# Second products of a gated MLP one slot later, in a fused attention + mixture-of-experts + MLP kernel on one core

## The reference

```python
x = _attn_ref(...)                      # 2 x 768 tokens, 512 channels, decayed linear attention
x = _moe_ref(x, domain_probs, w1, w2)   # 4 experts, 512 -> 1024 -> 512
def _moe2_ref(x, w_in, w_out):          # 1536 tokens, 512 -> 2048 -> 512
    h = x @ w_in
    g = h * np.cos(h)
    return (g @ w_out).astype(np.float32)
```

## Time and profile before

| | |
|---|---|
| median of 3 runs | 833.54 us (833.54 to 835.22) |
| the profiled execution, its own time | 833.52 us |
| its span | 831.6 us |
| PE busy | 804.2 us, 97% |
| DVE, ACT, POOL busy | 597.0, 334.4, 400.1 us |
| granted clock of TensorE, mean | 0.991 |
| MLP: first matmul (L1395) to the span's end | 539.0 to 831.6 us |

### The profile page before, as it was taken

How to read it: one execution, slowest core, us unless ns; L and a number is a source line. 1 busy time by engine, 2 the same in 40 slices (tenths; PEclk the granted TensorE clock), 3 DMA queues, 4 the chain that set the end, 5 groups by cost and what they waited for, 6 DMA issues and landing times.

```text
span 831.6 us, 11709 instructions
## 1 busy us (share of the span) xinstructions
PE 804.2 (97%) x4362; PEld 670.8 (81%) x4362; DVE 597.0 (72%) x924; ACT 334.4 (40%) x630; POOL 400.1 (48%) x357
## 2 busy tenths in 40 slices
PE   8999999999999999999999999979989989899898
PEld 7888888888888888888888888857867768677676
DVE  6887766766766766766766766687686776867796
ACT  4653222222222232232232232365757567575653
POOL 3976343343343343343343341547776667757631
PEclk9999999999999999999999999999999999999999
DMA  9931101121101111110110110001110101010003
GB/s 326 336 129 64 39 26 39 39 64 39 39 26 38 39 64 38 39 36 30 39 38 26 39 39 26 13 26 26 38 37 27 39 13 39 13 51 26 0 4 149
DMA packets 19868, 44.85 MB, mean 54 GB/s; under 512 B 2344, under 2 KB 2392, under 8 KB 19812
## 3 DMA queue, kind: packets, MB, share of 16 engines
q1 hardware_dynamic: 19812, 44.10, 16.3%
HBM read 40.93 MB, written 3.17 MB: 53 GB/s over the span
## 4 chain that ended last, share of the span: by engine, by line
PE 69%; DVE 14%; ACT 10%; issue 4%; DMA 1%; POOL 1%; SPq 0%; ACTq 0%; DVEq 0%
PE ps L1337 31%; PE ps L1318 27%; DVE temps L1185 5%; PE ps L1402 4%; DVE temps L1179 3%; PE ps L1395 2%; ACT temps L853 2%; ACT temps L834 2%; DVE temps L1131 1%; PE ps L1285 1%; PE ps L1235 1%; DMA att<-att_in 1%; DVE x_lo L995 1%; ACT ps L812 1%; ACT w_hi L664 1%
## 5 line engine op out<-in xcount | busy, mean ns | idle before, releaser
L553 POOL TENSOR_TENSOR h_lo<-temps,h_hi 128x512 fp32r<-128x512 f32 (+1 forms) x128 | 135.1, 1057 | 295.6 <-ACT h_hi L723 295.5
L723 ACT ACTIVATE h_hi<-temps 128x512 fp32r<-128x512 f32 (+1 forms) x128 | 67.2, 525 | 337.0 <-DVE temps L1007 337.0
L990 DVE TENSOR_TENSOR y<-ps,y 128x512 f32<-128x512 f32 x180 | 123.9, 689 | 71.8 <-PE ps L1337 71.8
L1337 PE MATMUL ps<-h_hi,w_hi 128*128 128x512 f32 x384 | 150.5, 392 | 0.1
L1318 PE MATMUL ps<-x_hi,w_hi 128*128 128x512 f32 (+1 forms) x448 | 150.5, 336 | 0.1
L1318 PE MATMUL ps<-x_hi,w_lo 128*128 128x512 f32 (+1 forms) x448 | 150.6, 336 | 0.0
L1318 PE MATMUL ps<-x_lo,w_hi 128*128 128x512 f32 (+1 forms) x448 | 150.5, 336 | 0.0
L1337 PE MATMUL ps<-h_lo,w_hi 128*128 128x512 f32 x384 | 150.4, 392 | 0.0
L1337 PE MATMUL ps<-h_hi,w_lo 128*128 128x512 f32 x384 | 149.4, 389 | 0.0
L603 POOL TENSOR_TENSOR x_lo<-temps,x_hi 128x512 fp32r<-128x512 f32 x54 | 73.1, 1364 | 52.1 <-ACT x_hi L789 51.8
L1318 PEld LDWEIGHTS ps<-x_hi,w_hi 128*128 128x128 f32 x448 | 84.7, 189 | 12.8 <-DVE temps L1002 0.3
(11 more groups left out here) (111 smaller groups left out, 1404.1 us busy)
## 6 DMA issues: line engine op xcount, KB each, us to landing
w_raw<-w_in SPq DMA_DIRECT2D x96, 256.0 KB, 2.7
att<-att_in SPq DMA_DIRECT2D x24, 512.0 KB, 7.0
temps<-p_scr SPq DMA_DIRECT2D x4, 768.0 KB, 4.2
out<-y SPq DMA_DIRECT2D x12, 256.0 KB, 2.1
att<-dp_in SPq DMA_DIRECT2D x1, 24.0 KB
p_scr<-att SPq DMA_DIRECT2D x1, 24.0 KB
lam<-lam_in SPq DMA_DIRECT2D x1, 6.0 KB, 1.6
```

The source lines that it names most:

```text
L553: pool.tensor_tensor(hs_lo[side][:, f, at], ring(s, i), f32(hs_hi[side][:, f, at]), ALU.subtract).then_inc(s_hlo, 1)
L723: act.activation(hs_hi[s % SIDES][:, f, at], ring(s, i), ACT.Copy).then_inc(s_hhi, 1)
L990: dve.tensor_tensor(at, from_bank, at, ALU.add).then_inc(s_y, 1)
L1337: mm = pe.matmul(ps[:, DOWN_BANK + g % DOWN_BANKS, :], ww[:, s // SIDES % 2, f, at], hh[side][:, f, tokens], start=(f == 0 and n == 0), st ...
```

## The change

The second products of quarters 0 to 6 move one slot later on TensorE, and VectorE's taking out of their results with them, since both read `mix`. Groups 0 to 3 now stand in slot 5, groups 4 and 5 in slot 0 of the next quarter, 6 to 9 in slot 1, 10 to 13 in slot 2, 14 and 15 in slot 3, 16 and 17 in slot 4. The last quarter's groups stay; groups 16 and 17 of quarter 6 come into part 0 of slot 46, which also has the first groups of the last quarter. ScalarE's carry-ins and carry-outs, its high of the sums (from quarter 1 on), and VectorE's combinations in the last quarter move one slot later too. GpSimd's low of T1 and of the second piece of the first weights come ahead of the sums' low. No instruction is added or removed.

```diff
 def mix(v, part):
-    if v < 4:
-        return 0, ()
-    m, t = (v - 4) // 6, (v - 4) % 6
-    return m, (MIX_LAST if m == FULL else MIX)[t][part]
+    groups = []
+    if v >= 5:
+        m, t = (v - 5) // 6, (v - 5) % 6
+        if m == FULL - 1 and t == 5:
+            groups += [(m, i) for i in ((16, 17) if part == 0 else ())]
+        elif m < FULL:
+            groups += [(m, i) for i in MIX[t][part]]
+    if v >= 6 * FULL + 4:
+        groups += [(FULL, i) for i in MIX_LAST[v - 6 * FULL - 4][part]]
+    return groups
...
                     gate_low(m, 1, 1)
+                    w1_low(q + 1, 1)
+                    token_low(m, 2, t2[0])
                     w2_sums_low(m)
-                    token_low(m, 2, t2[0])
-                w1_low(q + 1, 1)
...
-                if j == 1 and m:
+                if j == 2 and m:
                     carry_in(m - 1, 14)
-                if j == 2 and m:
+                if j == 3 and m:
                     carry_in(m - 1, 16)
...
                 elif j == 3:
                     sum_high(m, 2, 0)
-                    carry_out(m, 0)
-                    carry_out(m, 1)
                 elif j == 4:
                     gate_high(m, 3, 3)
                     sum_high(m, 4, 1)
+                    carry_out(m, 0)
+                    carry_out(m, 1)
...
-                if j == 1 and m:
+                if j == 2 and m:
                     carry_out(m - 1, 14)
-                if j == 2:
+                if j == 3:
                     if m:
                         carry_out(m - 1, 16)
                     carry_in(m, 0)
                     carry_in(m, 1)
                 if m < FULL:
-                    if j == (2 if m else 1):
+                    if j == (3 if m else 1):
                         w2_sums_high(m)
...
-                if m == FULL and j == 0:
+                if m == FULL and j == 1:
...
-                if m == FULL and j == 3:
+                if m == FULL and j == 4:
                     combined(5, second_sum(N5), second_sum(N5), second_sum(N7))
                     combined(6, second_sum(N3), second_sum(N3), second_sum(N6))
```

More of the change, by code:

```diff
@@ L1098, in second @@
             def second(v, part):
-                m, groups = mix(v, part)
-                for i in groups:
+                for m, i in mix(v, part):
                     if kept(m, i) or carried(m, i):
@@ L1412, in second @@
             def second(v, part):
-                m, groups = mix(v, part)
-                q = QUARTERS + m
-                for i in groups:
+                for m, i in mix(v, part):
+                    q = QUARTERS + m
                     if m == 0 and i == 0:
```

5 lines of the change are left out of this document (3 added, 2 removed).

## The result

| | before | after |
|---|---|---|
| median | 833.84 us (832.95 to 835.22, 18 runs) | 831.38 us (828.89 to 834.78, 18 runs) |
| ratio, 95% interval | | 0.997 (0.9961 to 0.998) |
| profiled execution, its span | 833.52, 831.6 us | 832.66, 830.7 us |
| granted clock, mean | 0.991 | 0.995 |
| last matmul starts | 828.12 | 827.27 |

823.1 was forecast with a range of 812.5 to 831.0; the time lies just above the range, and nearest to rival C (831.9).

What follows compares the result with a forecast made beforehand. The chain between ScalarE and VectorE was taken to set the MLP's pace. First quarter -5.3, five steady quarters -8.0, last stretch -0.8, end +2.7 and +1.0 gave -10.4 us: 823.1 us, range 812.5 to 831.

Steps and rivals of the forecast that it cites:

- rival C: Nothing gained: the pace doesn't depend on where the carried work stands; -1.6 us, 831.9 or above, chance 0.07.
- (a): Steady quarter, end of slot 2 to L834 of slot 3: two carry-ins and the sums' high leave, one carry-in comes, -1.5 us.
- (d): Slot 5, L834 to L853: one taking out less ahead of L1185, but L1185 probably meets a GpSimd low; -0.2 us.
- (f): Slot 2: group 13's taking out comes ahead of L1185, which waits for gate 1's low anyway; 0.
- (b): Slot 3, L834 to L853: L1185 would wait for T1's low on GpSimd; +0.4 us.
- (c): L853 of slot 3 to L853 of slot 4: a carry-out, two carry-ins and the sums' high come; +0.4 us.
- Term (e): Slots 0 and 1: carry-in gone -0.5, one taking out more +0.6, a carry-out gone -0.5; together -0.4 us.
- The first quarter: L834 of slot 3 of quarter 1 comes 5.3 us earlier, at 591.4; PE allows just that, nothing left over.
- The last stretch: Slot 3 of quarter 6 to slot 3 of the last: 32.3 us for PE and one stall, not 33.1; -0.8.
- The end: Slot 46 must make the 12 matmuls that slot 4 lost, +2.7 us; the later last two combinations cost +1.0.
- A: PE becomes the bound as L1185 moves off GpSimd's lows and collisions mostly vanish; -20.9 us, 812.6, chance 0.20.
- D: Slower: T4 and L1185 of slots 4, 5 and 0 wait for whole GpSimd operations; 836.1 us, chance 0.11.

Runs made afterwards that it cites:

- experiment 1: Changed kernel with a one-element GpSimd memset between gate 5's low and the second weights' low, quarters 0 to 6: 823.52 us, ratio 0.9885.
- experiment 3: Kernel before with one VectorE instruction ahead of L1185 in slot 0, quarters 1 to 7: one-element memset 834.74 us, 128-element memset 835.39, copy from PSUM 834.83.
- experiment 5: Changed kernel with GpSimd's old order: 825.38 us; second, kernel before with GpSimd's new order alone: 838.63; changed kernel with only T1's low behind the sums' low: 823.75.
- experiment 2: Changed kernel with the same one-element GpSimd memset one place later, behind the second weights' low: 831.43 us, ratio 0.9963.
- experiment 6: First, changed kernel with the last quarter's third and fourth combinations ahead of its first group's taking out: 831.09 us; second, all four combinations plus experiment 1's memset: 822.07.

## Why the prediction was wrong, step by step

**What bounds the kernel: right.** The chain sets the pace. Slot 2 to 3 lost 1.48 us (forecast 1.5) and TensorE found its banks earlier, but the quarter became only 0.3 shorter, as much as the chain gave. TensorE's idle time is still what the chain leaves over: 3.2 us a quarter (34.5 less 31.3), where 1.9 was forecast. The two smaller stalls that stood ahead of it are gone as forecast, and the one ahead of group 8, now in slot 1's product, is there, 1.5 us instead of 1.9; a new one waits for a carry-in, 0.60 at 727.12 (TensorE's timeline, quarter 5):

```profile
717.80 0.50 PE L1409 MATMUL ps<-x_hi,h_hi 128*128 128x512 f32 x1 [1.35 <-DVE y L1127]
```

**Terms (a) to (d) and (f): right.** For (b) L1192 was to meet T1's low: it does (699.63, 1.69 long, ending 0.55 after GpSimd's L610 of 699.48 and 1.29). For (c) L842 of slot 4 was to come 3.7 after L861 of slot 3 and L861 of slot 4 6.8 after it; they came 3.67 (701.35 to 705.02) and 6.84 (708.19) after. The sums' low was to start at 3.8: it started at 3.85 (705.20).

**Term (e): this is the step that failed.** "The carry-in ahead of L834 of slot 1 has gone, -0.5" is true, as the kernels in which the race is won show (4.33). But the term let L1185 of slot 0 keep its 0.67, and said nothing of whom it meets. It meets L592 or L599 within 10 ns. +0.63 was measured where -0.5 was forecast, 1.13 a quarter, and the rows have 1.15; the 7.9 us of experiment 1 are the seven quarters of it (7 x 1.15 = 8.1). Of the 8.2 us between forecast and account, 5.7 are in the five steady quarters, 1.2 in the last stretch (forecast -0.8, measured +1.1), and 0.9 in the first (2.4 won; 3.3 with the memset, 51.41 against 54.75 from the MLP's first L834). The rest, 2.0 in the first quarter, 0.7 in the last stretch and 0.3 at the end, is below.

**The steady quarters of before: a gain that was not in the forecast.** Against all this the forecast was too modest by 2.5 in the five quarters: it took 34.8 for each quarter of before, but two of them took 36.1, those in which L1185 of slot 0 had lost its race by 0.3. The windows say why (the granted clock is the number ahead of the DMA share), before and then after:

```profile
645.00:650.00 5.00, 4.73 (x14) 3.74 (x15) 4.53 (x8) 2.79 (x5) 3.23 (x3) 0.66 0.01 2
750.00:755.00 5.00, 4.07 (x12) 3.25 (x13) 4.53 (x8) 2.60 (x6) 3.56 (x3) 0.70 0.00 0
```

```profile
645.00:650.00 5.00, 3.61 (x16) 2.61 (x15) 3.92 (x7) 2.79 (x5) 4.48 (x4) 1.00 0.01 3
```

Before, TensorE stood still for 1.82 us until 645.27, and from 646.37 on made seven steps of 0.43 instead of 0.227: the lower of its two levels, 1.2 GHz. The result that VectorE takes out just ahead of L1185 came late by that:

```profile
650.60 0.69 DVE L1120 TENSOR_TENSOR h_f<-ps,h_f 128x512 f32<-128x512 f32 x1 [0.20 <-PE ps L1402]
```

In the five profiles with TensorE's order of before (the kernel before, the three of experiment 3 and the second of experiment 5) there are eleven such stretches of 0.43 us steps behind 570 us, and eleven races of slot 0 lost by 0.27 us or more, each just behind one of them. In the nine profiles with the changed order every window of 5 us from 570 to 810 us has a clock of 1.00. So 2.6 of the 4.9 us gained in these quarters are two accidents of the kernel before that have no counterpart after the change. The prediction did not have them; it read the 0.96 of the earlier trace rows, a window that holds the first of these falls, as the slow start of quarter 0. What in the change keeps the clock up is not shown; TensorE's longest stall of 590 to 800 us is 1.4 us after it, 1.8 before.

The rest of the five quarters is chance. They were put at -1.6 each where the terms add up to -1.3, 1.5 us in all; that came true because slots 3 to 5 of quarter 1 take 11.89 and not 12.67, and slot 5 to 0 is 0.12 shorter than by term (d). And experiment 1, where the race is won, lands at 823.5 beside the 823.1 forecast in part by luck: the 2.5 us from the clock make up for most of the 3.0 that the next three paragraphs miss.

**The first quarter: the wrong bound.** "PE allows just that ... nothing is left over" took TensorE for the bound: 28.6 us for 126 matmuls and 1.6 for the slow clock make 30.2, but from TensorE's restart to L842 of slot 3 it is 33.1 (562.53 to 595.61). TensorE was at its lower level for longer than before, nine steps of 0.43 us against six. Windows before, then after, the idle time ending at 561.16 and at 562.53:

```profile
560.00:565.00 5.00, 3.84 (x10) 3.04 (x11) 3.69 (x5) 1.32 (x3) 2.39 (x3) 0.57 0.00 0
565.00:570.00 5.00, 5.00 (x24) 4.14 (x23) 2.95 (x5) 3.62 (x6) 3.35 (x3) 1.00 0.44 105
```

```profile
560.00:565.00 5.00, 2.47 (x6) 1.99 (x7) 4.93 (x6) 2.09 (x4) 2.39 (x3) 0.53 0.00 0
565.00:570.00 5.00, 5.00 (x19) 4.02 (x18) 3.61 (x5) 3.39 (x6) 5.00 (x4) 0.78 0.18 52
```

But that is not why the stretch takes 33.1. Five kernels share it and lose its race (after, experiment 2, both changed kernels of experiment 5, and the first of experiment 6); they have 9, 8, 10, 7 and 6 slow steps, the step into group 8 behind them is 1.21, 1.56, 1.02, 1.65 and 1.79 us, the shorter the more slow steps there were, and the stretch takes 33.08 to 33.13 in all five. The chain is the bound here too, and by its steps it gave less than the prediction's list has:

| from slot to slot | counted on | measured |
|---|---|---|
| 3 to 5 of quarter 0 | -1.96, two waits of ScalarE | -1.33 |
| 5 to 0 | -0.2, (d) | -0.01 |
| 0 to 1 of quarter 1 | -0.5, (e) | +1.14, the race |
| 1 to 2 | -0.7, a wait for TensorE, and +0.1, (e) | -0.49 |
| 2 to 3 | -2.0 | -1.75 |

Term (e)'s carry-in could give nothing here: the kernel before has none in slot 1 of quarter 1, where slot 0 to 1 takes 4.33 already. The 1.6 for the slow clock was nearly right by luck: the slow steps before cost that, but the window it was worked out from is a later one.

**The last stretch: mis-sized.** Besides the race, slot 2 to 3 took 5.99 where before took 5.22: with the carry-ins in other places, ScalarE's L842 waited for the chain, not for TensorE, so that the 32.3 us that TensorE and one stall would need were not the bound (L842 of 801.45 has no wait, where L834 had 1.32).

**The end: right in kind, a little small.** The matmuls put back into slot 46 cost 2.5 (slot 45 to 46 takes 6.58, 4.08 before) where 2.7 was forecast, and L842 of slot 46 waits for TensorE, in ScalarE's timeline:

```profile
808.03 0.60 ACT L842 ACTIVATE temps<-ps 128x512 int32<-128x512 f32 x1 [2.68 <-PE ps L1402]
```

The combinations cost about 1.5 rather than 1.0 (4.0 less 2.5), with 0.99 and 0.39 of it in TensorE's stalls at 818.50 and 820.55.

**The rivals.** A (L1185 comes off GpSimd's lows) was the opposite of what happened: its mean rose. D named the right kind of mechanism, L1185 waiting for whole lows, but put it in slots 4, 5 and 0 together and priced it at up to 3 us a quarter; what was not in the terms happened in slot 0 alone, for 1.15. C gave nearly the right time by a reason that did not hold: the pace does depend on where the carried work stands. The Trainium skill's rule (SBUF — State Buffer, section Who interferes with whom), that issue order decides who blocks, was cited for slots 3 and 4 and agrees with the table of races: in the five rows without an instruction of mine on VectorE, the one that begins first is the one that isn't held up, down to 0.01 us. The rows of the 128-element memset and the copy don't go by the recorded starts of the two. I did not ask the rule of slot 0, where the order is the closest.

**What stays open.** Why GpSimd's low of gate 5 takes 1.27 to 1.28 after and 1.29 to 1.30 before, which is what turned the race, was not settled: both begin 1.17 after ScalarE's L842 or L834. Nor could VectorE be pushed back by hand, so that the theory rests on the GpSimd side (experiments 1 and 2) and on the table of races. Those show that who is first in slot 0 makes the 7.9 us; they do not show that recorded starts 0.01 us apart are the measure of it. Starts this close are not even an order in the records: with the one-element memset of experiment 3, L1187 is recorded at 686.76 and the memset, which stands ahead of it in VectorE's own list, at 686.78. And whether the memset of experiment 1 works as a delay of 0.03 us or by standing between two lows of GpSimd, these runs don't tell apart.

## What to carry to other kernels

Before costing an edit, list where VectorE's instructions on the chain begin close to one of GpSimd's: each such meeting is a coin with a price (here 1.15 us, seven times), and a forecast must hold both of its sides, as a range and not as a sum. Look whether all periods of the kernel before are alike: two of five here were 1.3 us longer, and the change won that without anyone having counted on it. When a change gives less than its terms, compare step by step around one period: steps that fit and one that doesn't name the cause faster than any busy share. And before a stretch is put down to one engine, see whether it gets longer when that engine gets slower; in the first quarter it did not.
